# Two mixtures of experts behind a gated attention: the next rows' turns and the list's products moved to the boundary between the two halves of an expert's output

## What is computed

```python
x = attention(q, k, v, a_re, a_im)            # (3072 tokens, 384)

# mixture 1: 8 experts, only for tokens with a positive skip score
do_compute = x @ w_skip > 0
e_idx = argmax(x @ w_gate); gate_w = softmax(...)[e_idx]
h = relu(x[mask] @ w1[e])                     # (tokens, 1024)
y[mask] = gate_w * (h @ w2[e])                # (tokens, 384)
x[do_compute] += y

# mixture 2: 8 other experts, all tokens, logits of normalised x and embeddings
out[mask] = gate_w * (relu(x[mask] @ w1[e]) @ w2[e])
```

## Time and profile before

| | us |
|---|---|
| median of 3 runs | 799.79 |
| the profiled execution | 799.45 |
| its span, first to last instruction | 797.5 |
| PE busy | 700.3 (88%) |
| DVE busy | 655.5 (82%) |
| ACT busy | 476.1 (60%) |
| POOL busy | 213.5 (27%) |
| stage of the mixtures' slots, first L1351 to the end of the span | 367.60 to 797.5 |

### The profile page before, as it was taken

How to read it: one execution, slowest core, us unless ns; L and a number is a source line. 1 busy time by engine, 2 the same in 40 slices (tenths; PEclk the granted TensorE clock), 3 DMA queues, 4 the chain that set the end, 5 groups by cost and what they waited for, 6 DMA issues and landing times.

```text
span 797.5 us, 17481 instructions
## 1 busy us (share of the span) xinstructions
PE 700.3 (88%) x6568; PEld 622.7 (78%) x6568; DVE 655.5 (82%) x1241; ACT 476.1 (60%) x660; POOL 213.5 (27%) x185
## 2 busy tenths in 40 slices
PE   0577786199999999948999999999999999999997
PEld 0323232188888888837999998998999999999997
DVE  7999999989999999966979767857897796676672
ACT  7869998667666766552566554646554545544541
POOL 3000001111111111005253566533334222243422
PEclk9889998589999999978999999999999999999999
DMA  7563732018843333457576766775575756756730
GB/s 194 164 207 126 246 126 107 14 52 148 168 118 118 105 94 117 148 106 217 183 252 201 251 214 208 262 221 192 202 237 174 252 188 205 245 200 186 251 135 30
DMA packets 90900, 136.85 MB, mean 172 GB/s; under 512 B 22474, under 2 KB 70070, under 8 KB 90656
## 3 DMA queue, kind: packets, MB, share of 16 engines
q1 hardware_dynamic: 83680, 119.54, 48.8%
q0 software_dynamic: 7168, 16.64, 5.9%
HBM read 124.15 MB, written 14.01 MB: 173 GB/s over the span
## 4 chain that ended last, share of the span: by engine, by line
PE 48%; DVE 4%; DMA 2%; issue 1%; ACT 1%; POOL 0%; POOLq 0%; SPq 0%; DVEq 0%
PE banks L1394 23%; PE banks L1351 22%; PE banks L1337 2%; DVE mix_spot L1587 1%; DVE w_lo L981 1%; DMA raw<-w1b 1%; DMA mix_rows<-xbuf,lists 1%; DVE mix_hT_lo L1686 0%; DMA xbuf<-mix_y,to_scatter 0%; PE banks L1329 0%; ACT mix_hT_hi L1434 0%; DVE mix_y L1710 0%; ACT w_hi L970 0%; POOL to_scatter L1227 0%; POOLq L1100 0%
## 5 line engine op out<-in xcount | busy, mean ns | idle before, releaser
L1351 PE MATMUL banks<-mix_xT_hi,w_hi 128*128 128x240 f32 x576 | 158.9, 276 | 0.6 <-DVE mix_xT_lo L1695 0.6
L1351 PE MATMUL banks<-mix_xT_lo,w_hi 128*128 128x240 f32 x576 | 158.8, 276 | 0.0
L1351 PE MATMUL banks<-mix_xT_hi,w_lo 128*128 128x240 f32 x576 | 158.7, 276 | 0.0
L1394 PE MATMUL banks<-w_hi,mix_hT_hi 128*128 128x384 f32 (+3 forms) x384 | 135.7, 353 | 3.7 <-DVE mix_hT_lo L1686 3.7
L1394 PE MATMUL banks<-w_lo,mix_hT_hi 128*128 128x384 f32 (+3 forms) x384 | 129.8, 338 | 0.0
L1394 PE MATMUL banks<-w_hi,mix_hT_lo 128*128 128x384 f32 (+3 forms) x384 | 129.8, 338 | 0.0
L1434 ACT ACTIVATE mix_hT_hi<-banks 128x480 fp32r<-128x480 f32 x96 | 54.7, 571 | 110.8 <-PE banks L1351 107.6
L1351 PEld LDWEIGHTS banks<-mix_xT_hi,w_hi 128*128 128x128 f32 x576 | 109.5, 190 | 0.9 <-issue 0.8
L1351 PEld LDWEIGHTS banks<-mix_xT_hi,w_lo 128*128 128x128 f32 x576 | 109.5, 190 | 0.0
L1351 PEld LDWEIGHTS banks<-mix_xT_lo,w_hi 128*128 128x128 f32 x576 | 109.5, 190 | 0.0
L1686 DVE SCALAR_TENSOR_TENSOR mix_hT_lo<-banks,mix_hT_hi 128x480 fp32r<-128x480 f32 x96 | 62.8, 655 | 50.1 <-ACT mix_hT_hi L1434 50.1
(11 more groups left out here) (230 smaller groups left out, 1430.5 us busy)
## 6 DMA issues: line engine op xcount, KB each, us to landing
raw<-w1b SPq DMA_DIRECT2D x16, 1536.0 KB, 7.6
raw<-w2b SPq DMA_DIRECT2D x16, 1536.0 KB, 6.6
A<-w2a_t SPq DMA_DIRECT2D x8, 1536.0 KB, 8.4
raw<-w1a SPq DMA_DIRECT2D x8, 1536.0 KB, 7.8
raw<-w2a SPq DMA_DIRECT2D x8, 1536.0 KB, 7.0
ring<-a SPq DMA_DIRECT2D x9, 864.0 KB, 5.1
qk<-q SPq DMA_DIRECT2D x48, 96.0 KB, 2.3
qk<-k SPq DMA_DIRECT2D x48, 96.0 KB, 2.3
```

Of the source, the lines that this page charges most:

```text
L1351: last = pe.matmul(pU[g % TURNS][:, n * N:(n + 1) * N], w1p[m][:, b, c, f * P:(f + 1) * P], xT[s][:, c, 0:N], start=(c == 0 and (s, m) == ...
L1394: last = pe.matmul(pD[0:m, half, 0:ph.width], hT[s][:, f, half * P:half * P + m], w2p[w][:, b, f, 0:ph.width], start=(f == 0 and (s, w) == ...
```

## The change

The six turns of a slot stand together at the end of the first half, behind its step 7, and the 24 products of the list behind them in one piece. In slot 15 the 24 products of `list_over` stand in one piece behind the last step of the second half. The turns wait for the gather of their rows and no more for y_ready. On ACT the high parts of both blocks of rows come before the two of w2. The semaphores of the scatters are now one for each buffer and block in place of one for each block, and the waits on them count accordingly.

```diff
-        self.scattered = [sem(f"scattered{s}") for s in range(SUB)]
+        self.scattered = [[sem(f"scattered{b}{s}") for s in range(SUB)] for b in range(2)]
...
-    TURNS_AT = ((0, 5), (1, 1))
...
-                        pool.wait_ge(ph.scattered[s], slot.j * 16)
+                        pool.wait_ge(ph.scattered[1 - slot.b][s], slot.i * 16 + 16 * slot.b)
...
-            def turn_next(before, nxt, s):
-                pe.wait_ge(nxt.ph.gathered[nxt.b][s], nxt.i * 16 + 16)
-                if before is not None:
-                    pe.wait_ge(before.ph.y_ready, before.j * SUB + (s + 1))
-                turn_x(nxt, s)
...
+            def turn_next(nxt):
+                for s in range(SUB):
+                    pe.wait_ge(nxt.ph.gathered[nxt.b][s], nxt.i * 16 + 16)
+                    turn_x(nxt, s)
+
+            def list_between(ph, slot):
+                if (ph.n, slot.at) == (0, "close0"):
+                    list_tokens(phases[1], 0, 2, ENTRY, listed, range(UNITS))
+                if (ph.n, slot.at) == (0, 2):
+                    list_over(ph, range(UNITS))
+                if (ph.n, slot.at) == (1, 0):
+                    list_tokens(phases[1], 2, 5, GATE, gated, range(UNITS))
+                if (ph.n, slot.at) == (1, 5):
+                    list_tokens(phases[2], 0, 5, ENTRY, listed, range(UNITS))
...
-                        if (half, f) in TURNS_AT and nxt is not None:
-                            turn_next(before, nxt, half)
-                        if half == 0:
-                            list_part(ph, slot, f)
-                        elif (ph.n, slot.at) == (1, 7) and f >= FC // 2:
-                            list_over(phases[2], range((f - FC // 2) * CHUNK, (f - FC // 2 + 1) * CHUNK))
+                    if half == 0:
+                        if nxt is not None:
+                            turn_next(nxt)
+                        list_between(ph, slot)
+                    elif (ph.n, slot.at) == (1, 7):
+                        list_over(phases[2], range(UNITS))
...
                     split_x(nxt, 0)
-                    if (ph.n, slot.at) == (0, 0):
-                        split_x(nxt, 1)
+                    split_x(nxt, 1)
                     weights.hi_part2(act, nxt, 0)
-                    if (ph.n, slot.at) != (0, 0):
-                        split_x(nxt, 1)
                     weights.hi_part2(act, nxt, 1)
...
-                    dve.wait_ge(oldest.ph.scattered[s], oldest.j * 16 + 16)
+                    dve.wait_ge(oldest.ph.scattered[oldest.b][s], oldest.i * 16 + 16)
```

More of the change, by code:

```diff
@@ L1201, in body @@
                 if ph.n == 1 and slot.at == 0:
-                    for s in range(SUB):
-                        sp.wait_ge(before.ph.scattered[s], before.j * 16 + 16)
+                    for done in before.ph.scattered[0] + before.ph.scattered[1]:
+                        sp.wait_ge(done, before.i * 16 + 16)
                         sp.sem_inc(weights.carrier, 1)
@@ L1209, in _ @@
             for ph in phases:
-                for s in range(SUB):
-                    sp.wait_ge(ph.scattered[s], tail.j * 16 + 16 if ph is tail.ph else 16 * E)
+                for done in ph.scattered[0] + ph.scattered[1]:
+                    sp.wait_ge(done, tail.i * 16 + 16 if ph is tail.ph else 8 * E)
                     sp.sem_inc(weights.carrier, 1)
@@ L1271, in scatter @@
                                             y[0:m, slot.b, s, 0:width], None,
-                                            bounds_check=NT - 1, oob_is_err=False).then_inc(ph.scattered[s], 16)
+                                            bounds_check=NT - 1, oob_is_err=False).then_inc(ph.scattered[slot.b][s], 16)
             def body(slot, before, oldest, nxt, later):
```

## The result

The changed kernel takes 803.24 us (median of 6 runs, 801.55 to 804.81), the kernel before beside it 798.74 us (6 runs): a ratio of 1.0059, 95% interval 1.0042 to 1.0077, or 4.7 us slower (4.5 by the medians). The forecast was 802.1 us, and the time lies in its range. But the sum behind it was +2.3 us, so about half of the loss is another thing than the forecast's.

A forecast was written before the change was run, and what follows sets the result against it. PE was taken to bound 21 of 24 slots, DVE or a load the first half of slots 6, 9 and 13. The terms gave +2.3 us on 799.45, so 801.8; the median, 0.3 higher, 802.1 us, range 798.5 to 804.6.

The forecast's parts named there:

- Turns: In all 23 slots with a next one, six turns in a row cost 0.66 us, as two groups do: nothing saved.
- The list: One piece instead of four saves 0.3 us per list where PE is the bound; 0.1 in slot 15.
- Slot 6: Step 6 still waits for DVE's fourth piece; turns and list now come behind that stall, paid in full: +1.0 us.
- Slot 13: Step 6 waits for DVE's fourth piece; three turns and an 80-column list lose their cover: +1.2 us.
- Slots 8 and 9: Three turns lose cover in slot 9, +0.3 us; slot 8's saved 0.3 becomes a longer stall there, worth nothing.
- Slot 11: With turns gone from ahead of step 6, PE arrives before DVE's fourth piece; a new stall costs +0.2 us.
- slot 3: Same DVE routing block as slot 11, but slot 2's turns come over 2 us earlier: 0, at most +0.3 us.
- The sum: Slot 2 -0.3, 6 +1.0, 8 and 9 +0.3, 11 +0.2, 13 +1.2, 15 -0.1: +2.3 us.
- The other edits: ACT's order, semaphores and dropped y_ready wait cost nothing; w2's low part moves 0.2 us or less, covered by next upper part.
- The clock: Rival, chance 0.08: longer idles ahead of steps 4 and 6 in slots 6, 9, 13 drop PE's clock, 1.7 us a dip.
- the prediction's own sign of being wrong: The forecast is wrong if PEclk shows a new dip, plain slots shrink, or step 6 of slots 6 and 13 comes earlier.
- Within 0.5%: Chance 0.85 that the changed kernel's time differs from before by no more than 0.5% (4 us).

The follow-up runs named there:

- the last experiment: Kernel without the three stalls, with turns and ScalarE's order as before the change and the list in one piece; 791.67 us, ratio 0.9916 to the kernel before.
- the routing run: Changed kernel with the routing table's load and its wait for the scatters moved from slot 8 to slot 9, behind w2's load; 797.12 us, ratio 1.0003.
- the filled run: Changed kernel with 11 and 7 extra identity turns ahead of steps 4 and 6 in slots 6, 9 and 13; 801.01 us, ratio 1.0032.
- the second measurement: The changed kernel again without an edit, beside other runs of the kernel before and with a second profile; 801.56 us, ratio 1.0047.
- the list alone: Against the kernel before, list in one piece as in the change, turns and ScalarE's order as before; 800.73 us, ratio 1.0027.
- the other edits: Against the kernel before, only the scatters' semaphores, the dropped y_ready wait and ScalarE's new order; turns and list as before; 799.39 us, ratio 1.0018.
- the turns alone: Against the kernel before, the six turns together as in the change, the list in pieces as before; 799.87 us, ratio 1.0021.

## Why the prediction was right, and where it was wrong

- **Turns: nothing. Right.** 0.65 us for six in a row, plain slots at 17.12 before and after, and no worth in the last experiment.
- **The list: 0.3 for each. Right.** Slot 8 fell by 0.31; slot 2 by 0.23 (18.84 to 18.61) and slot 15 by 0.17 (18.55 to 18.38), where -0.3 and -0.1 stood.
- **Slot 6: +1.0. Right,** 1.04, with step 6 at the same 14.02 us.
- **Slot 13: +1.2. Right,** 1.29 without the low clock (20.97 in the routing run, against 19.68).
- **Slots 8 and 9: +0.3. Right in kind; in size +0.3 to +0.55.** Without the low clock slot 9 is 20.23 in the filled run, 0.86 longer than before, so with slot 8 it is +0.55. But the stall's length differs between executions of one kernel. Step 6 of slot 9 begins 543.65 - 529.95 = 13.70 us into the slot in before, 14.23 in the first profile of the change, and in the second 542.19 - 528.15 = 14.04 (the line is shown with that run). That is 0.34 later, which is what slot 8 saved (18.12 to 17.78), and with three turns the forecast's +0.3. The reason for slot 9's stall was right and is shown by the routing run.
- **Slot 11: +0.2** measured 0.29; **slot 3: 0** measured 0.02.
- **The sum: +2.3.** The filled run has +2.8 in its slots and +2.6 in its median: the mechanism was right and the size about right.
- **The other edits: nothing. Nearly right for the change, and the reason was incomplete.** The 0.35 at the end of the program is in all eleven profiles with the change's semaphores and was in no term of the sum. For ScalarE's order the text named the upper part of the next slot as the cover. It did not see the routing block of DVE that stands behind the low part of w2 in slots 2 and 10, which has no such cover; the turns together made up for it. Left apart, these edits cost 1.4 us.
- **The clock: this step failed.** "In this trace the six short idles of slots 6, 9 and 13 left the clock at 1.00 and disagree with it" (with the rule that short idles can bring the clock down) took idle times of 1.14 us and less as a witness for idle times of 1.4 and 0.9 us in a row. That rival had a chance of 0.08. It came true with two falls in both profiles of the change, 4.3 us of the slots' 7.1 in the first and 2.6 of 5.5 in the second, and with it the prediction's own sign of being wrong, a new dip in PEclk. Its price of 1.7 us a dip, taken from slot 0, was near the 1.3 to 1.5 of a short fall. The first profile, the slowest of its six, has more of it than the median: by the medians the change costs 4.7 and 3.7 us, 2.6 of it exposed work with the end of the program, and 1.1 to 2.1 are left, as far as the profiles say for the clock. The filled run and the change were timed beside different runs of before, their intervals touch (up to 1.0044, from 1.0042 and 1.0031), and the medians alone do not prove the split; it rests on two profiles of the change and one of the filled run.
- **The range, 798.5 to 804.6, held in part by luck.** Its upper part was there for the scatter of the runs, and the falls of the clock, which it left out, happened to fit into it.
- **Within 0.5%, at 0.85:** the ratio is 1.0059 and in the second measurement 1.0047, on both sides of that bound.

## What to carry to other kernels

Small work on the bounding engine has no price of its own but that of its place: under a stall it is free, behind it it is paid in full. So before such work is gathered into one run, mark the stretches in which the engine waits, and leave it there, or remove the stall first: here that was worth 5 to 7 us, while gathering the work was worth nothing. When an edit empties a stall, count the idle time that it makes as a risk to TensorE's clock too. And an edit that is worth nothing beside another can cost by itself, as ScalarE's order did here: try the parts alone.

## What the runs showed of the hardware

- Two idle times of 1.4 and 0.9 us, 1.0 us of products apart, were followed by a granted clock of 0.50 for 3.4 or 6.8 us in four of six such places in two profiles of the change. Idle times of 1.14 and 0.58 us in before were not, nor 1.4 and 0.6 (slots 6 and 13 with the list alone, slot 9 with the other edits), nor 1.00 and 0.91 (slot 9 with the turns alone), in one profile each. Nor were the same 1.4 and 0.9 us in slots 6 and 13 of the one profile with the routing table later, so such idle time does not always do it. With transposes in them, which left at most 0.2 us, the clock was 1.00 in the profile.
- A fall of 3.4 us cost 1.3 to 1.5 us (slots 6, 9 and 13), one of 6.8 us 2.8 us (slot 9, first profile).
- Six fp32 transposes of 128 columns ran 0.11 us apart and 24 bf16 products of 32 columns 0.026 apart, and rows of two, three and five such transposes ran at the same 0.11.
